# Attention's q times kv of twelve token tiles: each head on 64 rows of the array, in place of block-diagonal head pairs

## The reference

```python
kv = np.einsum('bhsd,bhse->bhde', k, v)          # per batch and head, 64 x 64
out = np.einsum('bhsd,bhde->bhse', q, kv)        # 576 tokens x 64
rms = np.sqrt(np.mean(out * out, axis=-1, keepdims=True) + 1e-06)
attn = out / rms * g_norm                        # B, H, S, D = 4, 8, 576, 64
x = attn.transpose(0, 2, 1, 3).reshape(2304, 512)
x = (silu(x @ w_gate) * (x @ w_val)) @ w_out     # 512 -> 1536 -> 512
out = softplus(x @ w_in2) @ w_out2               # 512 -> 2048 -> 512
```

## Time and profile before

| | before |
|---|---|
| median of 3 runs | 886.56 us (886.12 to 887.71) |
| profiled execution | 886.71 us |
| its span in the trace | 884.9 us |
| PE busy, matmuls | 876.9 us, 5362 records |
| PE loads of weights | 814.6 us, 5362 records |
| DVE, ACT, POOL busy | 649.9, 440.5, 230.0 us |
| q times kv (line 912) | 120 matmul records, 67.9 to 184.0 us |
| k times v (line 905) | 240 matmul records, 49.3 to 152.2 us |

### The profile page before, as it was taken

The page is one execution under the profiler, slowest core; times in us unless marked ns, Lnnn a source line. Parts: engine busy times, 40 slices in busy tenths (PEclk is TensorE's granted clock), DMA queues, the critical chain, the costliest instruction groups (busy, mean ns, idle before and its releaser), DMA issues.

```text
span 884.9 us, 14699 instructions
## 1 busy us (share of the span) xinstructions
PE 876.9 (99%) x5362; PEld 814.6 (92%) x5362; DVE 649.9 (73%) x1254; ACT 440.5 (50%) x778; POOL 230.0 (26%) x189
## 2 busy tenths in 40 slices
PE   8999999999999999999999999999999999999998
PEld 7999999999999999999999998998998999999997
DVE  3655655788585877676777998878878878878875
ACT  4627454765342534342445764544554554554553
POOL 4643203599511399630255000000000000000000
PEclk9999999999999999999999999999999999999999
DMA  9985765542100022100033110000000000000100
GB/s 274 221 209 155 158 132 134 153 128 73 37 1 1 1 72 73 46 16 1 1 118 122 48 48 0 36 0 0 36 0 0 36 0 0 36 0 0 37 1 36
DMA packets 95541, 53.93 MB, mean 61 GB/s; under 512 B 37248, under 2 KB 86528, under 8 KB 95488
## 3 DMA queue, kind: packets, MB, share of 16 engines
q1 hardware_dynamic: 95328, 53.23, 22.3%
q10 hardware_dynamic: 160, 0.00, 0.0%
HBM read 44.96 MB, written 8.26 MB: 60 GB/s over the span
## 4 chain that ended last, share of the span: by engine, by line
PE 97%; DMA 1%; issue 1%; SPq 1%; ACT 0%; DVE 0%; POOL 0%; DVEq 0%; POOLq 0%
PE bank L972 23%; PE bank L974 23%; PE bank L973 23%; PE bank L1131 8%; PE bank L1130 7%; PE bank L1129 7%; PE bank L912 1%; PE bank L905 1%; PE bank L980 1%; PE bank L878 0%; PE bank L986 0%; DMA v_rest<-in_v 0%; PE bank L867 0%; DMA q<-in_q 0%; SPq L502 0%
## 5 line engine op out<-in xcount | busy, mean ns | idle before, releaser
L972 PE MATMUL bank<-x_hi,arena 128*128 128x384 f32 x554 | 187.0, 338 | 0.0
L974 PE MATMUL bank<-x_hi,arena 128*128 128x384 f32 x554 | 186.8, 337 | 0.0
L973 PE MATMUL bank<-x_lo,arena 128*128 128x384 f32 x554 | 186.0, 336 | 0.0
L972 PE MATMUL bank<-ring,slots 128*128 128x256 f32 x504 | 142.7, 283 | 0.3 <-DVE sum_b L1616 0.3
L974 PE MATMUL bank<-ring,slots 128*128 128x256 f32 x504 | 142.6, 283 | 0.0
L973 PE MATMUL bank<-ring,slots 128*128 128x256 f32 x504 | 142.6, 283 | 0.0
L1354 ACT ACTIVATE act_a<-bank 128x384 f32<-128x384 f32 x96 | 47.2, 492 | 173.9 <-PE bank L974 173.9
L1131 PE MATMUL bank<-arena,g_lo 128*128 128x512 f32 x288 | 113.1, 393 | 0.0
L1130 PE MATMUL bank<-arena,g_hi 128*128 128x512 f32 x288 | 112.9, 392 | 0.0
L1129 PE MATMUL bank<-arena,g_hi 128*128 128x512 f32 x288 | 111.9, 388 | 0.0
L972 PEld LDWEIGHTS bank<-x_hi,arena 128*128 128x128 f32 x554 | 104.4, 188 | 4.0
(11 more groups left out here) (140 smaller groups left out, 1657.5 us busy)
## 6 DMA issues: line engine op xcount, KB each, us to landing
stage<-in_moe_w_out SPq DMA_DIRECT2D x28, 256.0 KB, 3.5
out_dram<-out_stage SPq DMA_DIRECT2D x18, 256.0 KB, 2.1
k<-in_k SPq DMA_DIRECT2D x16, 256.0 KB, 3.3
v<-in_v SPq DMA_DIRECT2D x16, 256.0 KB, 3.3
stage<-in_moe_w_in SPq DMA_DIRECT2D x16, 256.0 KB, 2.8
xy<-in_q SPq DMA_DIRECT2D x48, 72.0 KB, 3.0
stage<-in_moe_w_gate SPq DMA_DIRECT2D x12, 256.0 KB, 3.7
stage<-in_moe_w_val SPq DMA_DIRECT2D x12, 256.0 KB, 4.1
```

Of the source, the lines that this page charges most:

```text
L972: nc.tensor.matmul(ps, hi, rhs_hi, start=first, stop=False)
L973: nc.tensor.matmul(ps, hi, rhs_lo, start=False, stop=False)
L974: return nc.tensor.matmul(ps, lo, rhs_hi, start=False, stop=last)
```

## The change

A list `APART` names twelve tiles: (1,0) to (1,3), (2,0) to (2,2) and all five of batch 3; eleven have 128 tokens and the last, (3,4), has 64. For these, `q_times_kv` takes each head by itself: 64 rows of `q_t` as the stationary side, the head's own 64 x 64 block of `kv_blocks` as the moving side. Even heads lie on rows 0 to 63 and go to bank `o_ps`, odd heads on rows 64 to 127 and go to bank `kv_ps`. The three other tiles, (1,4), (2,3) and (2,4), run in steps in which `kv_ps` collects the next batch's k times v, and keep their form.

As `kv_ps` now holds results of tiles, pair 0 of the next batch's k times v is moved from after the gate product to after the value product of its step, directly ahead of pair 1, and in batches 2 and 3 PE first waits there until the last apart tile of the batch before is multiplied. ACT squares a bank in one instruction each, so two of 256 columns per tile; DVE multiplies one bank per instruction, so two of 256 columns as before.

```diff
--- before.py
+++ after.py
@@ -120,6 +120,9 @@
 TILE_AT = {1: (6, 7, 8, 9, 10), 2: (12, 13, 14, 15, 16), 3: (17, 18, 19, 20, 21)}
 TILE_OF = {k: (b, j) for b in TILE_AT for j, k in enumerate(TILE_AT[b])}
 TURN_AFTER = 2
+
+
+APART = [(1, 0), (1, 1), (1, 2), (1, 3), (2, 0), (2, 1), (2, 2)] + [(3, j) for j in range(NT)]
 X_NEEDED = [0, NT + 2 - LATE0]
 X_NEEDED7 = [n - LATE0 for n in (2 * NT + 1, 3 * NT + 1, 4 * NT)]
 IDLE_PRODUCTS = (7, 2)
@@ -253,6 +256,7 @@
 
     gate_ps, val_ps, kv_ps, o_ps = bank[0], bank[1], bank[2], bank[3]
     acc_ps = bank[4:8]
+    apart_ps = [o_ps, kv_ps]
 
     hid_ps = bank[0:4]
 
@@ -908,6 +912,13 @@
 
         def q_times_kv(b, j, src, ps):
             pe.wait_ge(qt_ready, (b - 1) * NT + (j + 1))
+            if (b, j) in APART:
+                for t in range(KT):
+                    for odd, r in enumerate((slice(0, D), slice(D, P))):
+                        last = nc.tensor.matmul(apart_ps[odd][0:ROWS[j], t * D:(t + 1) * D], src[r, t, 0:ROWS[j]],
+                                                kv_blocks[r, t, r], start=True, stop=True)
+                last.then_inc(o_done, 1)
+                return
             for t in range(KT):
                 last = nc.tensor.matmul(ps[0:ROWS[j], t * P:(t + 1) * P], src[:, t, 0:ROWS[j]],
                                         kv_blocks[:, t, :], start=True, stop=True)
@@ -950,7 +961,6 @@
                 if k == KV_AT[b]:
                     if b == 1:
                         pe.wait_ge(x_ready, NLATE0)
-                    pair(b, 0)
                 if k == KV_AT[b] + 2:
                     pair(b, 2)
                     pair(b, 3)
@@ -959,6 +969,9 @@
 
             for b in range(1, B):
                 if k == KV_AT[b]:
+                    if b > 1:
+                        pe.wait_ge(xn_ready, tiles_before(b - 1) + len([x for x in APART if x[0] == b - 1]))
+                    pair(b, 0)
                     pair(b, 1)
             if k in TILE_OF:
                 b, j = TILE_OF[k]
@@ -1182,6 +1195,14 @@
             act.wait_ge(o_done, n + (j + 1))
             nc.scalar.activation(to[0:ROWS[j], :], src[0:ROWS[j], :], ACT.Square).then_inc(square_ready, 1)
 
+        def square_apart(n, j):
+            act.wait_ge(o_done, n + (j + 1))
+            r = slice(0, ROWS[j])
+            for odd in range(2):
+                last = nc.scalar.activation(squares[r, :].rearrange("s (t o d) -> s t o d", t=KT, o=2)[:, :, odd, :],
+                                            apart_ps[odd][r, 0:KT * D].rearrange("s (t d) -> s t d", t=KT), ACT.Square)
+            last.then_inc(square_ready, 1)
+
         def root(n, j):
 
             act.wait_ge(sum_ready, n + (j + 1))
@@ -1394,7 +1415,10 @@
                 x7_high(*EARLY_AT[k])
             if k in TILE_OF:
                 b, j = TILE_OF[k]
-                square_up(tiles_before(b), j, o_ps, squares)
+                if (b, j) in APART:
+                    square_apart(tiles_before(b), j)
+                else:
+                    square_up(tiles_before(b), j, o_ps, squares)
                 root(tiles_before(b), j)
             if k == 2:
                 for j in range(LATE0, NT):
@@ -1515,6 +1539,15 @@
             dve.wait_ge(inv_ready, n + (j + 1))
             if j >= 2 or b > 1:
                 dve.wait_ge(x_kept, kept_count(b, j - 2) if j >= 2 else kept_count(b - 1, NT - 2 + j))
+            if (b, j) in APART:
+                for odd in range(2):
+                    last = nc.vector.tensor_tensor(
+                        x_norm[number(b, j) % 2][r, :].rearrange("s (o u t d) -> s t o u d", o=2, u=2, t=KT)[:, :, odd, :, :],
+                        apart_ps[odd][r, 0:KT * D].rearrange("s (t u d) -> s t u d", t=KT, u=2),
+                        sums[r, 2, j, :].rearrange("s (t o u) -> s t o u", o=2, u=1)[:, :, odd:odd + 1, :].broadcast_to(
+                            (ROWS[j], KT, 2, BLK)), ALU.mult)
+                last.then_inc(xn_ready, 1)
+                return
             for half in range(2):
                 last = nc.vector.tensor_tensor(
                     x_norm[number(b, j) % 2][r, :].rearrange("s (o u t d) -> s t o u d", o=2, u=2, t=KT)[:, :, :, half, :],
```

## The result

| | before | changed |
|---|---|---|
| median | 886.51 us (7 runs) | 890.28 us (7 runs) |
| ratio | | 1.0041, 95% interval 1.003 to 1.0052 |
| profiled execution, its span | 886.71, 884.9 us | 890.57, 888.8 us |
| in a later series (after_again below) | 886.80 us (19 runs) | 889.17 us (10 runs), ratio 1.0029 (1.0019 to 1.0038) |

A forecast was written before the change was run, and what follows sets the result against it. PE's own stream was taken to bound the kernel. Full tiles +3.9, rest tile -0.4 and moved pair -0.6 sum to +2.9 us, giving a median of 889.5 us, range 884.5 to 892.5.

The forecast's parts named there:

- Part 1: Eleven full q times kv tiles on 64 rows: 1.59 us each instead of 1.235, in all +3.9 us.
- the bounds 0.06 and 0.222: Pair step of a full apart tile: 0.06 us if half the rows load twice as fast, 0.222 in turn; 0.112 taken.
- Part 2: Rest tile (3,4), apart as 8 pairs of 64 x 64: 1.17 us instead of 1.56, -0.4 us.
- Part 3: Pair 0 of k times v moved ahead of pair 1: 0.2 us saved per batch, three times, -0.6 us.
- The queue's delay: SP's queue in batch 2: the load of the next pair 2 and all behind it some 1.6 us late, cost taken at 0.
- PE's new wait for the normalised tiles: Ahead of pair 0 in batches 2 and 3: covered by 3.8 us, so no cost.
- Part 4: ACT's two squares cost it 0.2 us more per tile, DVE's multiplication stays two instructions; covered, so cost 0.
- Sum: Whole kernel: +3.9 - 0.4 - 0.6 = +2.9 us, a median of 889.5 us.
- B: Rival on full tiles: 64 rows load 128 columns twice as fast, pair step 0.06 us; 885.0 us, chance 0.11.
- D: Rival on full tiles: row halves don't load at once, +1.245 us per tile; 899.7 us, chance 0.13.
- C: Rival on full tiles: a change of rows between plain matmuls costs nothing, step 0.112 us; 885.7 us, chance 0.04.
- E: Rival: the forecast plus a lost cover, q blocks late or PE waiting at pair 0, +1 to +3 us; 892 us, chance 0.08.

The follow-up runs named there:

- after_again: The changed kernel, unedited, measured once more beside other kernels on one chip: 889.17 us, ratio 1.0029 to the kernel before.
- quarters: The changed kernel with each head's 128 tokens as two halves of 64 stationary columns, four 64 x 64 products at once: 886.32 us, ratio 0.9991.
- apart_twice: The changed kernel with each apart tile multiplied twice in a row, same operands and result, no further change of shape: 901.44 us, one run.

## Why the prediction was right

- **What bounds the kernel.** PE's stream: the large changes made on it came through, +0.45% for a change of shape in twelve tiles, 11 to 12 us over the changed kernel for the second multiplication (10.3 worked out, and 10.3 in the edited stretch less its wait and clock). The small ones are nearer to the noise. One reading was wrong without harm: the clock line of the page, read as full clock in all slices, hides a stretch of 3.4 us at half in its first slice of 22 us, which rounds to 9 tenths.
- **Part 1, the full tile.** 1.59 forecast, 1.59 measured, in its terms: 0.26 until the first load, an open load of 0.11, steps of 0.111 for 0.112, 0.43 from the last step on. The choice between the bounds 0.06 and 0.222 decided the forecast. It rested on two transposing loads of 138 and 140 ns; the plain ones came at 187 and 191. The Trainium skill's rule (TensorE: Matmul & The Clock Gate, section LDWEIGHTS: columns count, rows don't) holds here, by the 187 and 191 ns. The factor of up to two of the Trainium skill's page TensorEngine Tiling (Array Packing), section Theoretical Speedup, did not come with 64 rows alone, and came for the stream, 0.89 to about 0.47 us, when the loaded columns were halved too.
- **Part 2, the rest tile.** -0.4 forecast; 1.56 to 1.17.
- **Part 3, the move.** -0.6 forecast; 0.64 and 0.72 between the edited stretches with and without it, 0.57 between the medians on one chip. The queue's delay came as worked out, 1.4 to 1.7 us for 1.6 (in batch 1 step 8's weights were issued 2.1 us later, not 2.6), and PE waited for neither. PE's new wait for the normalised tiles appears among no waits.
- **Part 4, ACT and DVE.** 0 forecast; ratio 0.9996 for two squares alone. The second square costs ACT 0.06 us and not 0.2, which the cover hides either way.
- **Sum.** +2.9 forecast, +2.93 in the edited stretch of the profile. The medians say +3.6 (2.7 to 4.6) and +2.6 (1.7 to 3.4) us: the forecast lies in both intervals. The 0.8 us between the forecast of 889.5 and the first median is no larger than what the clock does to it. What the prediction did not see is outside the edit, where it expected an unchanged span: the first 45 us with their waits and clock (-1.3 to +1.3 us against the profile of before) and the start of the seven-product steps. In the profiled execution of the changed kernel these terms sum to +0.9; in its second one to -0.7, so that the exact +2.9 holds for the edited stretch and is partly luck for the whole.
- **Rivals.** B (step 0.06) and D (0.22) are refuted by the step of 0.111, C by the 0.25 us of idle time ahead of each tile, E by the waits.

## What to carry to other kernels

In this kernel a change of the array's shape costs about 0.35 us of PE for one excursion, in and out: gather the products of one shape, or don't leave it for work of under a microsecond. Before splitting a product by rows, ask whether the load or the moving side sets the step; here only splitting the loaded columns as well (64 by 64, four at once) shortened the stream, by half. And a PE-bound kernel can hold a DMA with no cover: the largest gain of this study came from fewer loaded columns together with two loads issued one place earlier, beside the moved pair: 0.38%, where quarters alone gave 0.09% in the median (0.2% at full clock) and the early loads alone nothing. Compare executions of one granted clock before reading a difference of 1 us.

## What the hardware showed that was not expected

One issue of a small DMA on SP's queue took 2.00 us where the same instruction takes 0.61, and its 1.4 us of delay went straight into PE's wait of 2.30. The granted clock falls to half after some waits of a microsecond and not after others: at 160 us in apart_twice after 1.30 us, as shown; in quarters after 2.30 us it stayed at 1.00. What decides it was not tried. And the same DVE instruction, 128 x 384, takes 1.0 or 1.5 us while POOL is busy beside it, within one kernel (0.98, 1.53 and 0.99 at 185.81, 192.51 and 198.07 us of before) and at one place in two; here it is in before and in the changed kernel, shortly ahead of the first seven-product step:

```profile
198.07 0.99 DVE L1581 TENSOR_TENSOR g_lo<-act_a,g_hi 128x384 fp32r<-128x384 f32 x1
```
```profile
201.72 1.54 DVE L1614 TENSOR_TENSOR g_lo<-act_a,g_hi 128x384 fp32r<-128x384 f32 x1
```

The 0.55 us between the two rows stands ahead of the first of the two waits for `sum_b`; PE is 0.34 us later behind it. That POOL's work next to it is the cause was not tried.
